# An attention, routing and expert kernel on one core: gate logits formed with the values, expert rows gathered by a table, and wider moving streams in the attention products

## The reference

```python
for t in range(S):
    kt, vt, rt = (k[:, :, t], v[:, :, t], r[:, :, t])
    cur = np.einsum('bhd,bhe->bhde', u[None] * kt, vt)
    y[:, :, t] = np.einsum('bhd,bhde->bhe', rt, state + cur)
    state = w[None, :, :, None] * state + np.einsum('bhd,bhe->bhde', kt, vt)
# x: (1536, 384), the heads side by side
logits = x @ w_gate                      # (1536, 8)
expert_idx = np.argmax(logits, axis=1)
# gate_w: the softmax of the chosen logit; slots are given in order of the tokens
h = np.maximum(np.einsum('ecd,edf->ecf', disp, w1), 0.0)   # F = 1024
y = np.einsum('ecf,efd->ecd', h, w2)
out[i] = gate_w[i] * y[expert_idx[i], pos[i]]
# dense layer, 384 -> 2048 -> 384
h = x @ w_in
return (h - np.tanh(h)) @ w_out
```

## Time and profile before

| | |
|---|---|
| median of 3 runs | 412.27 us (409.12 to 420.2) |
| the profiled execution, its own time | 410.51 us |
| its span, from the first to the last instruction | 408.8 us |
| busy, share of the span | PE 94%, PEld 91%, DVE 52%, ACT 44%, POOL 38% |
| mean granted TensorE clock, as a share of 2.4 GHz | 0.980 |

### The profile page before, as it was taken

How to read it: one execution, slowest core, us unless ns; L and a number is a source line. 1 busy time by engine, 2 the same in 40 slices (tenths; PEclk the granted TensorE clock), 3 DMA queues, 4 the chain that set the end, 5 groups by cost and what they waited for, 6 DMA issues and landing times.

```text
span 408.8 us, 10468 instructions
## 1 busy us (share of the span) xinstructions
PE 384.9 (94%) x3738; PEld 373.1 (91%) x3739; DVE 214.2 (52%) x453; ACT 180.9 (44%) x486; POOL 155.7 (38%) x132
## 2 busy tenths in 40 slices
PE   7999898698999999999999899999999999999991
PEld 7777687598999999999999899999999999999991
DVE  7667978574555655555465356615252434343340
ACT  5553456434564665756656454533022313231220
POOL 3966665435877742715517051541002000110002
PEclk9999999689999999999999999999999999999997
DMA  7989986444849478576684527000000000010001
GB/s 246 271 251 269 249 211 220 141 149 154 264 162 285 150 249 261 189 253 192 224 284 158 182 79 226 6 21 38 0 0 19 38 0 0 0 58 0 0 0 65
DMA packets 41541, 56.85 MB, mean 139 GB/s; under 512 B 3584, under 2 KB 39104, under 8 KB 41504
## 3 DMA queue, kind: packets, MB, share of 16 engines
q1 hardware_dynamic: 35936, 46.23, 36.9%
q10 hardware_dynamic: 3600, 5.31, 4.1%
q0 software_dynamic: 1968, 4.83, 3.1%
HBM read 46.23 MB, written 10.13 MB: 138 GB/s over the span
## 4 chain that ended last, share of the span: by engine, by line
PE 58%; issue 18%; POOL 13%; DVE 4%; DMA 2%; ACT 2%; another core or an unknown queue 1%; POOLq 0%; DVEq 0%; SPq 0%; ACTq 0%
POOL w_lo L460 11%; PE ring L1065 9%; PE ring L1067 9%; PE ring L1066 9%; PE pO L1317 8%; PE pO L1316 8%; PE pY L1189 2%; POOL token_of_rank L521 2%; PE ring L1205 2%; PE pA L1140 2%; PE pD L1094 1%; DVE At L880 1%; PE pY L1174 1%; PE pX L1084 1%
## 5 line engine op out<-in xcount | busy, mean ns | idle before, releaser
L460 POOL TENSOR_TENSOR w_lo<-raw_weights,w_hi 128x768 fp32r<-128x768 f32 x40 | 73.5, 1846 | 84.6 <-ACT w_hi L580 84.3
L1007 DVE SCALAR_TENSOR_TENSOR minus_tanh<-square,ring 128x384 f32<-128x384 f32 x64 | 35.5, 554 | 93.5 <-ACT square L730 79.1
L580 ACT ACTIVATE w_hi<-raw_weights 128x768 fp32r<-128x768 f32 x80 | 67.1, 848 | 28.5 <-DMA raw_weights<-w 28.4
L730 ACT ACTIVATE square<-ring 128x384 f32<-128x384 f32 x64 | 31.4, 491 | 94.7 <-DVE h_hi L1017 53.8
L1065 PE MATMUL ring<-yT_hi,w_hi 128*128 x192 | 65.0, 339 | 1.7 <-DVEq L1002 1.7
L1316 PE MATMUL pO<-w_hi,h_hi 128*128 128x384 f32 x192 | 64.9, 338 | 0.0
L1317 PE MATMUL pO<-w_lo,h_hi 128*128 128x384 f32 x192 | 64.8, 338 | 0.0
L1066 PE MATMUL ring<-yT_lo,w_hi 128*128 x192 | 64.8, 338 | 0.0
L1067 PE MATMUL ring<-yT_hi,w_lo 128*128 x192 | 64.8, 338 | 0.0
L1065 PE MATMUL ring<-xT_hi,w_hi 128*128 128x224 f32 x192 | 52.9, 275 | 1.6 <-issue 1.1
L849 DVE TENSOR_TENSOR w_lo<-raw_weights,w_hi 128x768 fp32r<-128x768 f32 x40 | 42.4, 1073 | 22.3 <-ACT w_hi L580 18.7
(11 more groups left out here) (158 smaller groups left out, 744.1 us busy)
## 6 DMA issues: line engine op xcount, KB each, us to landing
raw_weights<-w SPq DMA_DIRECT2D x80, 384.0 KB
x_by_slot<-x ACTq DMA_DIRECT2D x9, 576.0 KB, 4.4
x_expert<-x_by_slot SPq DMA_DIRECT2D x8, 576.0 KB
kv<-kv_by_token SPq DMA_DIRECT2D x22, 192.0 KB, 4.2
rkT<-rk_by_feature SPq DMA_DIRECT2D x18, 192.0 KB, 5.1
rkT<-rk_by_feature SPq DMA_DIRECT2D x3, 512.0 KB, 4.5
x_expert<-x_by_slot SPq DMA_DIRECT2D x1, 384.0 KB
x_by_slot<-x,sloti POOLq DMA_INDIRECT x12, 4.1
```

Of the source, the lines that this page charges most:

```text
L460: pool.tensor_tensor(lo, unit_raw(2, k), hi.bitcast(F32), ALU.subtract).then_inc(w2_ready, 1)
L580: act.activation(hi, unit_raw(what, k), ACT.Copy).then_inc(w1_hi if what == 1 else w2_hi, 1)
L730: act.activation(sq[:, i % 2, :], ring[i % 4][:, 0:CAP], ACT.Square, scale=THIRD ** 0.5, accum_out=sqsum[:, bass.ds(t * (2 * FC) + i, 1)]) ...
L1007: dve.scalar_tensor_tensor(out=nt[:, i % 2, :], in0=sq[:, i % 2, :], scalar=1.0, in1=ring[i % 4][:, 0:CAP], op0=ALU.subtract, op1=ALU.mult ...
```

## The change

**Logits with the values.** v is now loaded by feature too (`rkvT`, half as large again as `rkT`). PE multiplies it by the gate's weights of each head beside the own products (four more matmuls with a weight of 18 columns); the transpose that was there for the diagonal carries the result, and ACT's new `gated_values` writes it behind each head's 48 values, so that a head has DV = 56 columns. State, `vdiag` and `pY` carry them along; `route1` sums the 8 heads' shares with one DVE reduction. The three transposes of x, their copy and the logit products and copies go.

**Wider streams.** The 64x64 score products of the second half stream 128 columns instead of 64, and the products that streamed 48 columns stream 64, some of them not read.

**Rows by a table.** x goes to DRAM by token, in plain stores from SP's queue. DVE's `places_of` and POOL's `spread` make one-hot factors, PE multiplies them into a table of the token at each slot (`tabled`, once for steps 0 to 7 and once for 8 to 11), and POOL gathers each expert's rows with three indirect DMAs. The clearing and the scatters go. `route1` moves to steps 4, 8, 10 and after the loop, `route2` to 5 and 9 and after; DVE's `low` of expert 0's first weights moves from steps 10 and 11 to behind the routing.

```diff
-                last = pe.matmul(pA[keys, par, p, HALF:P], kw[rows, d, 1, p, :], rwq[rows, d, p, 2, :],
+                last = pe.matmul(pA[keys, par, p, :], kw[rows, d, 1, p, :],
+                                 rwq[rows, d, p, 1:3, :].rearrange("p b t -> p (b t)"),
...
-                last = pe.matmul(pX[32 * p:32 * p + 2, D:D + P], ucol[:, p, :], rkf[:, p, :], start=True, stop=True,
-                                 skip_group_check=True)
+                pe.matmul(pX[32 * p:32 * p + 2 * E + 2, D:D + P], own_gate[:, 0, p, :], rkf[:, p, :],
+                          start=True, stop=False, skip_group_check=True)
+            pe.wait_ge(feature_in[n % 3], loaded_features(n))
+            for p in range(NP):
+                last = pe.matmul(pX[32 * p:32 * p + 2 * E + 2, D:D + P], own_gate[:, 1, p, :], rkT[:, n % 3, 2, p, :],
+                                 start=False, stop=True, skip_group_check=True)
...
             pe.wait_ge(value_in[s], 16 * (n // 3 + 1))
+            pe.wait_ge(vg_ready, n + 1)
...
-            if n > 0:
-                x_transposed(n - 1)
...
-            if n > 0:
-                logits(n - 1)
...
+            def gated_values(n):
+                act.wait_ge(dg_full, n + 1)
+                act.wait_ge(value_in[n % 3], 16 * (n // 3 + 1))
+                act.copy(vg[:, n % 3].rearrange("p (a b) e -> p a b e", b=2)[:, :, :, DH:DV],
...
+                    decayed_state(n + 1)
+                    gated_values(n + 1)
+                    diagonals(n + 1)
...
-                dve.wait_ge(lg_done, first + m)
+                dve.wait_ge(x_ready, first + m)
+                gated = x[:, first % XS:first % XS + m, :].rearrange("p i (h e) -> p i e h", h=H)
+                link(dve.tensor_reduce(logit[:, 0:m], gated[:, :, DH:DV, :], AX.X, ALU.add))
...
+            def places_of(g, link):
+                first, m = GROUPS[g]
+                tiles = slice(first, first + m)
+                link(dve.tensor_tensor(allf[:, 2, tiles], allf[:, 1, tiles], limit[:, tiles], ALU.is_lt))
+                link(dve.copy_predicated(tokslot[:, tiles], allf[:, 2, tiles].bitcast(U32), allf[:, 1, tiles]))
+                link(dve.tensor_tensor(past[:, 0:m], bc(tokslot[:, tiles].unsqueeze(2), [P, m, Q + 1]),
+                                       bc(bounds[:, :].unsqueeze(1), [P, m, Q + 1]), ALU.is_ge))
+                link(dve.tensor_reduce(reached[:, tiles], past[:, 0:m], AX.X, ALU.add))
+                dve.scalar_tensor_tensor(out=lane_no[:, tiles], in0=reached[:, tiles], scalar=float(P),
+                                         in1=tokslot[:, tiles], op0=ALU.mult, op1=ALU.subtract).then_inc(places_ready, 1)
...
+            def spread(g):
+                pool.wait_ge(places_ready, g + 1)
+                if g == 2:
+                    pool.wait_ge(table_full, 1)
+                first, m = GROUPS[g]
+                for n in range(first, first + m):
+                    pool.tensor_scalar(qhot[:, n % DIRECT, :], counts[:, :], reached[:, n:n + 1], None, ALU.is_equal)
+                    last = pool.tensor_scalar(phot[:, n % DIRECT, :], lanes[:, :], lane_no[:, n:n + 1], tokno[:, n:n + 1],
+                                              ALU.is_equal, ALU.mult)
+                last.then_inc(hot_ready, 1)
...
-            sp.dma_start(xe[:, :, :], expert_rows(1)).then_inc(xe_in, 16)
...
+            for n in range(STEPS):
+                sp.wait_ge(xg_ready, n + 1)
+                sp.dma_start(x_d[1 + n * P:1 + (n + 1) * P, :], row(n)).then_inc(stored[n], 16)
+            for k in range(4):
+                unit(2, 0, k)
...
+            def expert_rows(e):
+                pool.tensor_copy(row3[:, :], row_i[:, e, :]).then_inc(row3_made, 1)
+                pool.wait_ge(row3_made, e)
+                for k in range(BLOCKS):
+                    gather(x_d, row3, k, xe_in)
...
+            tabled(range(DIRECT), 2)
+            pe.wait_ge(x_ready, STEPS)
             for c in range(KD):
                 direct(8, c, near, True, False)
...
+            keep_warm(4, ones[:, :], pT[:, 0, :])
...
+            pe.wait_ge(table_done, 1)
+            tabled(range(DIRECT, STEPS), NG)
...
+                pool.wait_ge(ring_full, e * RING + (RING + KD))
+                expert_rows(e + 2)
```

More of the change, by code:

```diff
@@ L622, in decayed_state, with table_copy @@
                     last.then_inc(stw_ready, 1)
+            def table_copy(g):
+                act.wait_ge(table_full, g + 1)
+                act.copy(table[:, g, :], pD[:, 0:Q]).then_inc(table_done, 1)
             def decayed_queries(n):
@@ L910, in _ @@
             spots_of(11)
-            rows_of(2)
-            rows_of(3)
+            places_of(2, rlink)
+            places_of(3, rlink)
+            low(0, 0, 0)
             link = chained(dve, m_c)
@@ L1125, in positions, with tabled @@
                           start=False, stop=True).then_inc(pos_full, 1)
+            def tabled(tiles, hot):
+                pe.wait_ge(hot_ready, hot)
+                for n in tiles:
+                    last = pe.matmul(pD[:, 0:Q], phot[:, n % DIRECT, :], qhot[:, n % DIRECT, :], start=(n == tiles[0]),
+                                     stop=(n == tiles[-1]))
+                last.then_inc(table_full, 1)
             for n in range(STEPS):
@@ L1164, in _ @@
                             h = 2 * p + par
-                            last = pe.matmul(pT[rows, p, 0:DH], kend[:, d, p, par, :], kv[:, s, 1, DH * h:DH * (h + 1)],
+                            values, shift = stream(vg[:, s].rearrange("p h e -> p (h e)"), h, H)
+                            last = pe.matmul(tflat[rows, p * P + shift:p * P + shift + WIDE], kend[:, d, p, par, :], values,
                                              start=True, stop=True, skip_group_check=True)
@@ L1173, in _ @@
                             for par, rows in enumerate(halves):
-                                pe.matmul(pY[t, par, DH * p:DH * (p + 1)], rwq[rows, d, p, half, :], st[rows, d, p, :],
+                                state, shift = stream(st[rows, d].rearrange("p a e -> p (a e)"), p, NP)
+                                pe.matmul(pY[t, par, WIDE * p + shift:WIDE * (p + 1) + shift], rwq[rows, d, p, half, :], state,
                                           start=(p == 0), stop=False, skip_group_check=True)
```

342 lines of the change are left out of this document (169 added, 173 removed).

## The result

The changed kernel takes 424.75 us (median of 4 runs, 423.48 to 427.44), the kernel before beside it 411.45 (4 runs, 409.12 to 420.2). The ratio is 1.035, its interval 1.027 to 1.044: 3 to 4% slower, where 406.5 was forecast and 416 was the upper end of the range. The profiled execution took 427.44 us, its span 425.7.

The account below looks back on a forecast made before the run. PE's products were taken to bound experts and dense layer, narrowly also plain loop steps. Span 408.8 + 1.1 - 3.2 - 3.3 + 1.0 = 404.4, 406.1 with 1.7 around it; 406.5 us given, 400 to 416 at eight in ten.

Parts of the forecast that it names:

- 0.7 us of instruction gaps: Loop from P(0) to P(11): a fixed 0.7 us added once for gaps in PE's instructions.
- A plain step: Loop step without routing: PE's work falls from 4.94 to 4.14 us, 4.2 taken for each of five steps.
- rival B: Loop: the wide streams aren't free, 0.42 to 1.0 us in some seven steps, 409.5 to 413 us; chance 0.13.
- steps with `route2` or `places_of`: Loop: five more DVE instructions, 1.1 us, giving 4.65, 4.95 and 4.95 us for P(5), P(6) and P(9).
- `vg_ready`: Loop: a new wait of PE's growth products for ACT's `gated_values`, 2.2 to 2.8 us after `At`.
- Start: Ahead of the loop: larger first load 0.8 us, gate products 0.33; P(0) at 14.5 instead of 13.4, loss 1.1.
- P(11) to the first expert: Behind the loop: PE's chain of 14.2 us decides, plus 2.5 for half clock; 16.7 against 20.0, gain 3.3.
- The half clock: Between P(11) and the first expert: each us of work at half clock costs another; 2.5 us taken.
- Experts: Experts 0 to 2: POOL falls behind by some 2 us twice; cost 1.0 us, between 0 and 2.5.
- rival D: Experts: late gathers or POOL's backlog make PE wait in every expert, one us each, 414 us; chance 0.08.
- Rival C: Loop: PE's clock falls during waits behind `route1`; light form 409 to 411 us, heavy 418 to 422; chance 0.14.
- All three signs of being wrong: Plain step above 4.6 us; first expert before 84 or after 91; last 316 us growing by more than 3.

Follow-up runs that it names:

- e14: e1 (light loads, partly stale data) plus nine warming products on PE behind each of the three routing steps; loop 57.4 us, gaps 0.6.
- e3: Changed kernel with no column streamed that isn't read; 426.69 us, ratio 1.040.
- e1: Changed kernel with feature, key and value loads cut to 128 columns from step 3 on, partly stale data; loop 58.3 us, gaps 1.7.
- e17: Changed kernel with the values' features loaded as a transfer of their own behind each step's key rows, same bytes; 426.33 us, ratio 1.037.
- e8: Changed kernel with the edits of e4, e5, e6 and e7 together; 424.39 us.
- e18: Changed kernel with edits of e4, e6, e7, e9 (scatters only), e14's warming, twelve warming products before the early rows, e17's cut; 411.15 us, ratio 1.003.
- e9: Changed kernel with the third early gather ahead of the last two spreads and twelve scatters moved out of experts 0 and 1; 421.34 us, ratio 1.024.
- e5: Changed kernel with the third early gather ahead of the last spreads, and next-expert gathers ahead of the scatters in experts 0 and 1; 426.03 us.
- e6: Changed kernel with another order behind the loop: warming products, then step 8's direct products, then the table; 426.65 us.
- e4: Changed kernel with the state products of both query halves in one, sixteen records fewer a step; 423.69 us, ratio 1.034.
- e7: Changed kernel with the first feature load in two, the values' part later with its own semaphore; 428.42 us.
- e13: Changed kernel without the values' share of the feature loads from step 3 on, stale values; loop 60.3 us, gaps 1.2.
- e10: Kernel before with one more load of 256 KB a step from step 3 on, into an unread buffer; 411.19 us, ratio 0.993.

## Why the prediction was wrong

The span was forecast at 404.4 us and is 425.7. Of these 21.3 us the loop has 8.1, the stretch behind it 6.2, the experts 5.6 and the start 1.4. Without the loop's 8.1 the median, 424.75, would still be 416.7, above the range.

The step that failed first is the one that put 0.7 us of instruction gaps on the whole loop. They were 11.0. The kernel before showed 2.7 us of them in its own loop, and the prediction gives no reason why a shorter step should have fewer: it treats the gaps as a small fixed addition and not as a limit that a shorter step would meet. PE must get one block of 256 instructions in about each step, and the round of a fetch, 5.0 to 6.4 us here, is longer than the 4.4 us that the block lasts. With the gaps away (e14) the loop is 57.4, to a forecast of 56.3; with them 64.4.

The other parts of the loop stood in the main. A plain step was forecast at 4.14 for PE and 4.2 in all; in e14 the first four take 4.18, 4.25, 4.56 and 4.18 (the one from P(7) 4.80). Widening was taken as free: e3 shows it, and rival B is out: four side-by-side tiles still take 0.11 us. The 134 cycles for 128 columns that the Trainium skill gives ("TensorE: Matmul & The Clock Gate", Back-to-back issue gap) don't add up over such tiles. Gate products 0.33: 0.34. P(4) and P(8) at 6.9: 6.58 and 6.95. Of the steps with `route2` or `places_of`, set at 4.65, 4.95 and 4.95, two were too short and one too long (e14: 5.34, 5.59 and 4.36), and P(10) took 6.64 for 6.2. `vg_ready`, to which the prediction had PE's waits put down, is named by no wait of PE in the changed kernel, e1 or e14.

Start: forecast 14.5, measured 15.88. The term for the larger first load, 0.8, was too small; DVE starts at 6.19, 1.2 us behind what was 4.96, and the first products, behind a wait of 2.56 us for the queries, run at half clock (8.7 to 12.1 us), which the forecast had at nothing. e17 and e8 reach 13.8 and 13.6.

P(11) to the first expert: 16.7 forecast, 22.9 measured. The half clock was forecast at 2.5 us for a part of the stretch and lasts 13.6 of 23 us, up to 6.8 by the prediction's own rule; a wait of 2.23 for `lane_hot` was left out. (DVE's terms there add up to 12.9 and not 12.8, which changes nothing.) With both mended (e18) it is 18.9.

Experts: 1.0 forecast, 0 to 2.5 allowed, 6.6 measured. The prediction lets POOL fall behind "by some 2 us twice", but takes its price from `w2_ready` and the weight loads, not from the gathers that stand behind the scatters; those it leaves to rival D, at 0.08. PE waited 1.08 and 2.81 for rows and 0.81 for `h_lo`, and lost about 2 to the clock. POOL's backlog was right, the place where it is paid wrong; e9 settles it.

Rival C, at 0.14, shows itself where the gaps leave PE early enough at the wait for `x`. Its fall of the clock behind step 4 is absent in the changed kernel, e5 and e6, with 11.0, 8.3 and 9.0 us of gaps, and present in e1, e3, e4, e7, e8, e9, e13 and e17, with 1.2 to 5.3. All three signs of being wrong came true: plain steps of 4.98 to 6.36 us, the first expert at 103.2, and 6.6 more in the last stretch.

## What to carry to other kernels

Before shortening a stretch of straight-line code on PE, look for "issue" gaps inside a group of products that carry no wait of their own, and for whether they move by a fixed number of records: there instruction supply is the next limit, and time taken off PE's work goes into the gaps as long as the number of instructions stays. Count instructions and not only time, warming products included. Where a serial engine's queue (POOL here) gets more work than a period has, moving the parts around only changes who waits; take work that nobody needs yet out of the crowded periods. A single profile of such a loop scatters by 3 us, so read a remedy from its own stage and from many runs.

## What the runs showed of the hardware

The long gaps of PE lie a multiple of 256 instructions apart (one count is 255), matmuls, weight loads and the sequencer's together, and PE went on 2.2 to 3.0 us after the start of the packet of 16 KB on its instruction queue, in eight gaps out of eight. With light loads (e1) the first five packets come 3.9 to 4.3 us apart, and there is no gap before 52 us. The loads act on the time ahead of the packet: in the changed kernel the next one stood 2.2 us behind the first gap's end, in e1 1.1 behind the same matmul. What lets them delay the fetch is open: without the values' features the gaps were 1.2 us and not 5 to 11 (e13), 256 KB a step more, at 273 GB/s, brought the kernel before only from 2.7 to 4.3 (e10), and the cut of the transfers (e17) moved them within the scatter. The granted clock did not fall at once when PE went idle, but 1.9 to 2.9 us later (e8: idle from 36.35 to 38.56, half clock from 39.2; e3: idle from 22.69 to 25.09, half clock from 24.6), so its price fell on the products behind the wait.
